# Diagonal values and state decays of three units move from GpSimd to ScalarE, and three transposes change their step

## The chip, the cores and the metric

The kernel runs on one core of a Trainium2 chip. The metric is the device time of one execution in microseconds (us), and less is better. The kernel has five instruction streams of its own: TensorE (PE), VectorE (DVE), ScalarE (ACT), GpSimd (POOL) and SyncE (SP), which issues all DMAs. Every stream runs in program order, and the streams meet at semaphores only.

## What is computed

Three layers follow one another on the tensors of four sequences (B = 4) of 768 tokens and eight heads of 48 values:

```python
# 1. attention with a decaying state
for t in range(S):
    cur = np.einsum('bhd,bhe->bhde', u[None] * kt, vt)
    y[:, :, t] = np.einsum('bhd,bhde->bhe', rt, state + cur)
    state = wt[:, :, :, None] * state + np.einsum('bhd,bhe->bhde', kt, vt)
# 2. gated MLP, 384 -> 2048 -> 384
h = x @ w_in
g = h * np.clip(h + 3.0, 0.0, 6.0) / 6.0
x = g @ w_out
# 3. soft mixture of 8 experts with 4 slots each
logits = x @ phi
d = softmax of logits over the tokens; slot_input = d.T @ x
slot_out = max(slot_input @ w1, 0) @ w2, for each expert
out = (softmax of logits over the slots) @ slot_out
```

The term `u * k * v * r` of a token with itself is the diagonal: for each head, the sum of r·u·k over its 48 values is one number for each token, and the token's v is multiplied by it.

## The kernel before

**Units and steps.** The attention is cut into 24 units: unit n is block n // 4 of 128 tokens of sequence n % 4. Units are counted from zero. The MLP is cut into 96 steps: step s = 16 g + i computes the hidden tile i (128 of the 2048 hidden values) for group g of 512 tokens (one block of all four sequences). Units 0 to 3 are computed before step 0. From then on the loop `for s in range(END)` stands in each of the five streams, and four steps go with one unit: `unit_of(s)` gives the unit n and the phase 0 to 3 of step s. Step 4 is phase 3 of unit 5, step 8 phase 3 of unit 6, step 12 phase 3 of unit 7.

**One MLP step.** TensorE multiplies the tile (nine matmuls, lines 617 to 619) into one of two PSUM banks. ScalarE makes the relu (line 1474) and VectorE the gated tile (`gate`, line 1076) and its transpose (`turn_gated`, line 1097), which goes into a ring buffer. Step s of TensorE waits for the gated tile of step s - 2, as it overwrites its bank. Every four gated tiles, TensorE adds their logits (line 665). After 16 of them, the logits of a group are folded (`low_logits` on VectorE, line 1105, then lines 696 and 697 on TensorE), their maximum is taken (line 1111), ScalarE makes weights of them (line 1499), VectorE turns these (line 1142), and in phase 2 of i = 3 of the next group TensorE gathers the slots from the ring (`gather_slots`, line 728). VectorE adds these to the accumulator at i = 4 (`add_slots`, line 1166). `turn_logits(g)` (line 1120, four small transposes) copies the folded logits of group g to the place where they are needed near the end.

**One unit.** Phase 0: TensorE makes the scores (line 501); GpSimd multiplies r, k and u (lines 1641, 1643); VectorE finishes y of the unit before (`finish_y`, line 1036, which adds the diagonal values) and adds to its state (line 1045). Phase 1: TensorE turns x (line 600); VectorE masks the scores (line 1017), then scans the decays of the next unit (lines 985, 997, and 963, 976 from unit 8 on); ScalarE splits the masked scores (`high_scores`, line 1381) and GpSimd makes their low half (`low_scores`, line 1676). Phase 2: VectorE makes the low half of x (line 1049), sums the diagonal (line 1056) and, for units 4 to 7, makes the low half of v (`low_v`, line 1060). Phase 3: TensorE computes y of the unit (`attend`; its first matmul has line 576 for units 4 to 7), which waits for the low halves of scores, v and x and for the decayed state. For units 8 and up, GpSimd makes the low half of v, and ScalarE decays the state (`decay_new_state`, line 1410).

**What the change touches.** `diag_values(n)` on GpSimd (line 1670) multiplies v by the diagonal, after it come `decay_state(n + 1)` (line 1712, for units 4 to 7) and `low_state` (line 1705). Both signal others: `finish_y` of the unit waits for `diag_v_done`, `attend` for `decayed`. In steps 1, 2, 5, 6, 9 and 10 GpSimd also makes low halves of w_in (`low_w`, line 1655), for which ScalarE makes the high half and a scaled copy (lines 1446 and 1452) in steps 0, 4, 5, 8 and 9, behind the relu of the step.

Of the kernel before, what the change touches and what calls it, by code (L numbers as in the profile page):

```python
# [50 lines left out]
def build_program(nc, wT, rkT, nat_in_dram, u, u_blocks, w_in, w_outT, w_out, phi, w1, w2, out):  # L51
    with ExitStack() as ctx:
# [900 lines left out]
        def _(dve):  # L953
# [269 lines left out]
            for s in range(END):  # L1223
                n, phase = unit_of(s)
                g, i = divmod(s, FT)
                if s <= 1:
                    gate(s)
                    if s == 0:
                        low_v(B)
                    turn_gated(s)  # L1230
                if phase == 0:
                    if 1 <= g < C and i == 1:
                        low_logits(g - 1)
                    if is_unit(n - 1):
                        finish_y(n - 1)
                    if n - 1 < LAST_INC:
                        add_state(n - 1)
                    if 1 <= g < C - 2 and i == 9:
                        turn_logits(g - 1)
                if phase == 1:  # L1240
                    if 1 <= g < C and i == 2:
                        group_maximum(g - 1)
                    if is_unit(n):
                        mask_scores(n)
                    if n + 1 < SPLIT:
                        scan_suffix(n + 1)
                        restart_prefix(n + 1)
                    elif is_unit(n + 1):
                        open_prefix(n + 1)
                        restart_suffix(n + 1)  # L1250
                    if is_unit(n - 1) and n % B == 0 and n > B:
                        low_x(n - 1)
                    if 1 <= g < C and i == 2:
                        if g == C - 1:
                            turn_gated(s - 1)
                        turn_weight(g - 1)
                    if g == C and i == 2:
                        last_maximum()
                if phase == 2:
                    if g == C and i == 3:  # L1260
                        turn_weight(C - 1)
                    if g >= 1 and i == 3:
                        sum_weight(g - 1)
                    if is_unit(n - 1) and n % B:
                        low_x(n - 1)
                    if is_unit(n):
                        sum_diag(n)
                    if n < SPLIT:
                        low_v(n)
                if s == 0:  # L1270
                    sum_diag(B)
                    low_w(1)
                if phase == 3:
                    if B < n and n + 1 < SPLIT:
                        scan_prefix(n + 1)
                    elif B < n and is_unit(n + 1):
                        close_suffix(n + 1)
                    if s == STEPS + 4:
                        dve.wait_ge(run_sum_done, C)
                        nc.vector.tensor_scalar(run_sum, run_sum, 1e-9, None, ALU.add).then_inc(sum_inv_step, 1)  # L1280
                        dve.wait_ge(sum_inv_step, 1)
                        nc.vector.reciprocal(run_sum, run_sum).then_inc(sum_inv_step, 1)
                        dve.wait_ge(sum_inv_step, 2)
                        nc.vector.tensor_scalar(fold_inv[:], fold32, run_sum, None, ALU.mult).then_inc(fold_inv_done, 1)
                        dve.wait_ge(fold_inv_done, 1)
                        nc.vector.tensor_scalar(fold_alpha, fold_inv[:], alpha, None, ALU.mult).then_inc(fold_inv_done, 1)
                    if 1 <= g < C and i == 4:
                        if g == C - 1:
                            turn_logits(g - 1)
                        add_slots(g - 1)  # L1290
                if s == 4:
                    dve.wait_ge(w_phi_ready, 4)
                    nc.vector.transpose(w_phi[:], l_ps[:]).then_inc(w_phi_done, 1)
                if s == STEPS - 12:
                    cols, tiles = c_parts[0]
                    dve.wait_ge(logits_done, C - 1)
                    nc.vector.tensor_reduce(cmax[:, tiles], by_slot(soft[:, cols]), AX_X, ALU.max).then_inc(c_max_done, 1)
                if s == STEPS - 8:
                    c_inverse(0)
                if s == STEPS + 3:  # L1300
                    copy_cT(1)
                    copy_cT(0)
                if 1 < s < STEPS - 1:
                    gate(s)
                if s == STEPS - FT - 1:
                    turn_logits(C - 3)
                if 1 < s < STEPS - 2 and s != STEPS - FT + 1:
                    turn_gated(s)
                if s == STEPS - 1:
                    last_gate(0)  # L1310
                    turn_gated(STEPS - 2)
                    last_gate(1)
                    turn_gated(STEPS - 1)
# [52 lines left out]
        def _(act):  # L1366
# [38 lines left out]
            def decay_new_state(n):  # L1405
                act.wait_ge(decay_saved, n - SPLIT + 1)
                act.wait_ge(state_added, n - B + 1)
                for p in range(PB):
                    s = state[n % B][0:PD, p, :]
                    last = nc.scalar.activation(s, s, ACT.Copy, scale=chunk_decay[n % B][0:PD, p:p + 1])  # L1410
                last.then_inc(decayed, 1)

            def high_receptance(n):
                act.wait_ge(r_dec_done, n + 1)
# [3 lines left out]
            def high_state(n):  # L1418
                if n < SPLIT:
                    act.wait_ge(state_added, n - B + 1)  # L1420
                else:
                    act.wait_ge(decayed, n - B + 1)
                    act.wait_ge(y_ready, n + 1)
                nc.scalar.activation(state_hi[n % B][0:PD], state[n % B][0:PD], ACT.Copy).then_inc(state_hi_done, 1)
# [129 lines left out]
            for s in range(END):  # L1554
                n, phase = unit_of(s)
                g, i = divmod(s, FT)
                if phase == 0:
                    if g >= 1 and i == 1:
                        copy_logit_parts(g - 1)
                    if is_unit(n):  # L1560
                        high_v(n)
                        if n >= SPLIT:
                            high_receptance(n)
                if phase == 1:
                    if is_unit(n - 1):
                        high_x(n - 1)
                    if 1 <= g < C and i == 2:
                        weigh(g - 1)
                        copy_folded(g - 1)
                    if is_unit(n):  # L1570
                        high_scores(n)
                if phase == 2:
                    if n < LAST_INC:
                        copy_keys(n)
                    if SPLIT <= n + 1 < UNITS:
                        save_decay(n + 1)
                    if SPLIT - B <= n - 2 < LAST_INC:
                        high_state(n - 2)
                if phase == 3 and SPLIT <= n - 1 < LAST_INC:
                    decay_new_state(n - 1)  # L1580
                if s < STEPS - 1:
                    relu_step(s)
                elif s == STEPS - 1:
                    for half in range(2):
                        last_relu(half)
                if s == 0:
                    copy_keys(B)
                c = scaled_behind(s)
                if c is not None:
                    high_w(c)  # L1590
                    scale_w(c)
                if g == C and i == 2:
                    weigh(C - 1)
                    copy_logits(C - 1)
                if s == STEPS - 10:
                    c_exp(0)
                if s == STEPS - 5:
                    c_high(0)
# [35 lines left out]
        def _(pool):  # L1634
# [110 lines left out]
            for s in range(END):  # L1745
# [15 lines left out]
                if phase == 3:  # L1761
                    if B < n and n + 1 < SPLIT:
                        decay_receptance(n + 1)
                    elif B < n and n + 1 < UNITS:
                        decay_keys(n + 1)
                    if is_unit(n) and n > B:
                        diag_values(n)
                    if n + 1 < SPLIT:
                        decay_state(n + 1)
                    if SPLIT - B <= n - 2 < LAST_INC:  # L1770
                        low_state(n - 2)
                c = split_behind(s)
# [75 lines left out]
```

## Time and profile before

| | |
|---|---|
| median of three runs | 410.31 us (410.25 to 410.34) |
| the profiled execution | 410.12 us, of which the span from first to last instruction is 408.4 us |
| mean granted TensorE clock | 0.992 of full speed |
| MLP steps 0 to 95 | from 35.7 us to some 352 us of the span |

The times of all rows are counted from the start of the span. In a timeline each row is one or several instructions: its start, its duration, engine, line, operation, what it writes and reads, the shape and how many; in square brackets how long the engine stood idle before and which instruction ended that. TensorE's instructions are pipelined, so a row of 0.38 us is followed by the next after 0.22 us.

### The profile page before, as it was taken

The numbers are of one execution on the slowest core, as the hardware profiler recorded it, in microseconds if no ns is written. First come the engines' busy times: TensorE is split into PE (matmuls) and PEld (weight loads), VectorE is DVE, ScalarE is ACT, GpSimd is POOL, SyncE is SP. The second block draws the span as 40 slices with busy tenths as digits, with TensorE's granted clock in tenths as the row PEclk, the third lists the DMA queues.
The fourth block names the chain that finished last, engine by engine and source line by source line (L and its number), as shares of the span: only waits on it lengthen the run. The fifth ranks groups of instructions, "written<-read, shape, count | busy, mean of one in ns | idle before, by whom it ended". The sixth has DMA issues, their size and how long they took to land.

```text
span 408.4 us, 10082 instructions
## 1 busy us (share of the span) xinstructions
PE 391.8 (96%) x3977; PEld 210.4 (52%) x3977; DVE 330.9 (81%) x536; ACT 199.8 (49%) x413; POOL 217.5 (53%) x206
## 2 busy tenths in 40 slices
PE   8999999999999999999999999999999999999981
PEld 3885555555555555555554555455543444543430
DVE  7998799998989898998989998989877886661251
ACT  3576356545555657365555646653443234321141
POOL 2444988978568677747785677875740012010000
PEclk9999999999999999999999999999999999999996
DMA  8999413439242144214431330342007199779929
GB/s 235 332 405 324 143 31 98 125 123 362 80 127 82 48 125 129 93 38 125 126 103 28 127 117 24 114 128 59 2 2 309 21 414 400 240 285 414 388 113 354
DMA packets 16542, 69.36 MB, mean 170 GB/s; under 512 B 2160, under 2 KB 3184, under 8 KB 14832
## 3 DMA queue, kind: packets, MB, share of 16 engines
q1 hardware_dynamic: 16496, 68.73, 48.6%
q8 instruction: 31, 0.51, 0.5%
q14 instruction: 15, 0.12, 0.1%
HBM read 64.00 MB, written 4.72 MB: 168 GB/s over the span
## 4 chain that ended last, share of the span: by engine, by line
PE 29%; POOL 29%; issue 27%; DMA 5%; DVE 4%; ACT 1%; SPq 1%; POOLq 0%; DVEq 0%
DMA att<-rkT_dram 5%; PE hid L617 4%; POOL att L1697 4%; PE hid L619 4%; PE hid L618 4%; POOL att L1641 4%; POOL att L1643 4%; POOL att L1670 3%; POOL att L1701 3%; POOL spare L1705 3%; PE hid L887 3%; POOL att L1662 3%; POOL w_split L1655 2%; PE inc_ps L728 1%; POOL att L1685 1%
## 5 line engine op out<-in xcount | busy, mean ns | idle before, releaser
L617 PE MATMUL hid<-x_split,w_split 128*128 128x512 f16 x285 | 108.3, 380 | 0.7 <-DVE gated L1076 0.7
L1474 ACT ACTIVATE relu<-hid,three 128x512 f32<-128x512 f32 x95 | 65.0, 684 | 88.1 <-PE hid L619 88.1
L619 PE MATMUL hid<-x_split,w_split 128*128 128x512 f16 x285 | 108.0, 379 | 0.0
L618 PE MATMUL hid<-x_split,w_split 128*128 128x512 f16 x285 | 108.0, 379 | 0.0
L1076 DVE SCALAR_TENSOR_TENSOR gated<-relu,hid 128x512 f32<-128x512 f32 x95 | 64.2, 676 | 21.5 <-ACT relu L1474 21.1
L1097 DVE STREAM_TRANSPOSE ring<-gated 128x512 f32<-128x512 f32 x96 | 68.3, 711 | 3.3
L1676 POOL TENSOR_TENSOR att<-att 128x1024 f16<-128x1024 f32 x20 | 42.1, 2104 | 34.9 <-ACT att L1381 34.9
L617 PEld LDWEIGHTS hid<-x_split,w_split 128*128 128x128 f16 x285 | 27.7, 97 | 37.1 <-issue 7.1
L619 PEld LDWEIGHTS hid<-x_split,w_split 128*128 128x128 f16 x285 | 27.8, 98 | 33.7
L1685 POOL TENSOR_TENSOR att<-att 112x512 f32<-112x512 f32 x21 | 25.5, 1213 | 36.5 <-DVE att L976 26.9
L618 PEld LDWEIGHTS hid<-x_split,w_split 128*128 128x128 f16 x285 | 27.9, 98 | 24.7
L1430 ACT ACTIVATE x_split<-y_ps 128x384 f16<-128x384 f32 x24 | 11.8, 490 | 39.8 <-PE y_ps L600 39.8
L501 PEld LDWEIGHTS sc_ps<-att 48*128 48x128 f32 x384 | 23.3, 187 | 9.3 <-issue 7.0
L501 PE MATMUL sc_ps<-att 48*128 48x128 f32 x384 | 27.9, 284 | 0.0
L1381 ACT ACTIVATE att<-att 128x1024 f16<-128x1024 f32 x20 | 21.1, 1056 | 12.6 <-DVE att L1017 11.6
L728 PE MATMUL sc_ps<-ring,soft 32*32 32x512 f32 x384 | 26.1, 598 | 0.0
L728 PE MATMUL k_ps<-ring,soft 32*32 32x512 f32 x192 | 25.7, 598 | 0.0
L1697 POOL TENSOR_TENSOR att<-att 112x512 f32<-112x512 f32 x19 | 23.5, 1235 | 3.0 <-DVE att L997 3.0
L1017 DVE TENSOR_TENSOR att<-sc_ps,mask 128x1024 f32<-128x1024 f32 x19 | 22.7, 1194 | 0.5 <-issue 0.5
L963 DVE TENSOR_TENSOR_SCAN att<-att 112x517 f32<-112x517 f32 x16 | 22.2, 1388 | 0.0
L1643 POOL TENSOR_TENSOR att<-att 128x384 f32<-128x384 f32 x20 | 20.9, 1043 | 1.6
L665 PE MATMUL l_ps<-gated,w_phi 128*32 128x512 f32 x160 | 21.3, 605 | 0.0
(300 smaller groups left out, 862.3 us busy)
## 6 DMA issues: line engine op xcount, KB each, us to landing
att<-nat_dram SPq DMA_DIRECT2D x20, 576.0 KB, 4.3
att<-rkT_dram SPq DMA_DIRECT2D x22, 448.0 KB, 5.7
att<-wT_dram SPq DMA_DIRECT2D x22, 226.2 KB, 4.7
att<-w_dram SPq DMA_DIRECT2D x3, 1536.0 KB, 9.7
out_dram<-w_split SPq DMA_DIRECT2D x11, 384.0 KB, 3.9
att<-w_dram SPq DMA_DIRECT2D x5, 768.0 KB, 10.5
stage<-w_in_dram SPq DMA_DIRECT2D x2, 1536.0 KB, 14.6
ring<-w_outT_dram SPq DMA_DIRECT2D x1, 3072.0 KB, 16.6
```

The lines of the kernel that those rows point to most:

```text
L501: last = pe.matmul(sc_bank[j][:, cols], k_dec[n % 2][rows, cols], r_dec_of(n)[rows, cols], start=True, stop=True)
L617: pe.matmul(hid[s % 2][:], high, x_high, start=(q == 0), stop=False)
L618: pe.matmul(hid[s % 2][:], high, x_low, start=False, stop=False)
L619: last = pe.matmul(hid[s % 2][:], low, x_high, start=False, stop=(q == KT - 1))
L728: ins = pe.matmul(dg_bank_of(g, a)[SLOTS * c:SLOTS * (c + 1), :], weight_T[SLOTS * a:SLOTS * (a + 1), b * SLOTS:(b + 1) * SLOTS], ring_gro ...
L1076: nc.vector.scalar_tensor_tensor(gated_tile(s), relu_tile(s), 6.0 * GATE, hid[s % 2][:], ALU.min, ALU.mult).then_inc(gated_done, 1)
L1097: nc.vector.transpose(ring_tile(s), gated_tile(s)).then_inc(gated_turned, 1)
L1474: nc.scalar.activation(relu_tile(s), hid[s % 2][:], ACT.Relu, bias=three[:], scale=GATE / H_SCALE)\
L1643: nc.gpsimd.tensor_tensor(rku, rku, u_all, ALU.mult).then_inc(rku_done, 1)
L1676: nc.gpsimd.tensor_tensor(scores_lo, scores, scores_hi, ALU.subtract).then_inc(scores_lo_done, 1)
L1685: nc.gpsimd.tensor_tensor(dst, keys, decay, ALU.mult).then_inc(k_dec_done, 1)
L1697: nc.gpsimd.tensor_tensor(dst, receptance, decay, ALU.mult).then_inc(r_dec_done, 1)
```

## The change

ScalarE gets two functions. `decay_old_state(n)` multiplies the state by the decay in four instructions, one for each pair of heads; it stands ahead of the relu of steps 0, 4 and 8, for units 5, 6 and 7. `loop_diag_values(n)` makes the diagonal values in eight instructions, one for each head; it stands behind the relu of steps 4, 8 and 12, for units 5, 6 and 7. GpSimd no longer does either for these units, one instruction each. Unit 4 stays on GpSimd, and the diagonal values of units 8 and up as well.

On VectorE three things move. `turn_logits(2)` runs in step 53 instead of step 57. `turn_gated(80)` runs at its place behind `gate(80)` no more, but in step 82, where `turn_gated(81)` stood; `turn_gated(81)` runs at the head of phase 2 of step 83.

```diff
@@ VectorE
-                    if 1 <= g < C - 2 and i == 9:
+                    if (g, i) in ((1, 9), (2, 9), (3, 5)):
                         turn_logits(g - 1)
...
                     if 1 <= g < C and i == 2:
                         if g == C - 1:
-                            turn_gated(s - 1)
+                            turn_gated(s - 2)
                         turn_weight(g - 1)
...
                 if phase == 2:
+                    if s == STEPS - FT + 3:
+                        turn_gated(s - 2)
...
-                if 1 < s < STEPS - 2 and s != STEPS - FT + 1:
+                if 1 < s < STEPS - 2 and s not in (STEPS - FT, STEPS - FT + 1):
                     turn_gated(s)
@@ ScalarE
+            def decay_old_state(n):
+                act.wait_ge(suffix_done, n + 1)
+                act.wait_ge(state_copied, n - B + 1)
+                for p in range(PB):
+                    s = state[n % B][0:PD, p, :]
+                    first = 1 + p * (P + 1)
+                    last = nc.scalar.activation(s, s, ACT.Copy, scale=suffix[0:PD, first:first + 1])
+                last.then_inc(decayed, 1)
+
+            def loop_diag_values(n):
+                act.wait_ge(diag_done, n + 1)
+                act.wait_ge(y_done, n)
+                if n >= SPLIT:
+                    act.wait_ge(v_scaled, n - SPLIT + 1)
+                for h in range(H):
+                    cols = slice(h * D, (h + 1) * D)
+                    last = nc.scalar.activation(diag_v[:, cols], nat_of(n, 2)[:, cols], ACT.Copy, scale=diag[:, h:h + 1])
+                last.then_inc(diag_v_done, 1)
...
+                if phase == 3 and n + 1 < SPLIT:
+                    decay_old_state(n + 1)
                 if phase == 3 and SPLIT <= n - 1 < LAST_INC:
                     decay_new_state(n - 1)
                 if s < STEPS - 1:
...
                 if s == 0:
                     copy_keys(B)
+                if phase == 3 and B < n < SPLIT:
+                    loop_diag_values(n)
@@ GpSimd
-                    if is_unit(n) and n > B:
+                    if is_unit(n) and n >= SPLIT:
                         diag_values(n)
-                    if n + 1 < SPLIT:
-                        decay_state(n + 1)
```

## Rows read from the trace of the kernel before

**Rows 1.** The page, part 1: busy time, share and instructions.

```profile
PE 391.8 (96%) x3977; PEld 210.4 (52%) x3977; DVE 330.9 (81%) x536; ACT 199.8 (49%) x413; POOL 217.5 (53%) x206
```

**Rows 2.** The waits: who waited for whom; us, times, longest.

```profile
DVE att L1036 <- POOL att L1670: 7.5, 11, 0.8
```

**Rows 3.** The timeline of TensorE, steps 4, 8 and 12 with their attends.

```profile
52.79 0.39 PE L617 MATMUL hid<-x_split,w_split 128*128 128x512 f16 x1
...
56.40 0.38 PE L617 MATMUL hid<-x_split,w_split 128*128 128x512 f16 x1
...
68.46 0.43 PE L576 MATMUL y_ps<-att 112*128 112x96 f32 x2 [0.47 <-DVE att L1060]
...
80.00 0.38 PE L617 MATMUL hid<-x_split,w_split 128*128 128x512 f16 x1 [0.27 <-DVE gated L1076]
...
83.11 0.43 PE L576 MATMUL y_ps<-att 112*128 112x96 f32 x2 [1.01 <-DVE att L1060]
...
84.83 0.38 PE L617 MATMUL hid<-x_split,w_split 128*128 128x512 f16 x1
```

**Rows 4.** The timeline of VectorE, steps 5 to 12, and a scan of step 22.

```profile
59.89 0.68 DVE L1076 SCALAR_TENSOR_TENSOR gated<-relu,hid 128x512 f32<-128x512 f32 x1
...
62.35 2.05 DVE L985 TENSOR_TENSOR_SCAN att<-att 112x517 f32<-112x517 f32 x1
...
66.76 1.44 DVE L1060 SCALAR_TENSOR_TENSOR att<-att 128x384 f16<-128x384 f32 x1
...
72.79 0.56 DVE L1036 SCALAR_TENSOR_TENSOR att<-y_ps,att 128x384 f32<-128x384 f32 x1 [0.81 <-POOL att L1670]
...
73.72 0.68 DVE L1076 SCALAR_TENSOR_TENSOR gated<-relu,hid 128x512 f32<-128x512 f32 x1
...
76.32 2.73 DVE L963 TENSOR_TENSOR_SCAN att<-att 112x517 f32<-112x517 f32 x1
...
79.18 0.67 DVE L1076 SCALAR_TENSOR_TENSOR gated<-relu,hid 128x512 f32<-128x512 f32 x1
...
120.30 1.21 DVE L963 TENSOR_TENSOR_SCAN att<-att 112x517 f32<-112x517 f32 x1
```

**Rows 5.** ScalarE: two groups by line and shape, relus of steps 5 and 9, split scores.

```profile
L1410 ACT ACTIVATE att<-att,stats 112x96 f32<-112x96 f32 x48 | 14.0, 372 | 0.0
L1469 ACT ACTIVATE att<-soft,diag 128x48 f32<-128x48 f32 x8 | 1.9, 323 | 0.0
...
58.54 0.69 ACT L1474 ACTIVATE relu<-hid,three 128x512 f32<-128x512 f32 x1 [0.89 <-PE hid L619]
...
72.33 0.69 ACT L1474 ACTIVATE relu<-hid,three 128x512 f32<-128x512 f32 x1 [1.59 <-PE hid L619]
...
76.30 1.06 ACT L1381 ACTIVATE att<-att 128x1024 f16<-128x1024 f32 x1 [0.92 <-DVE att L1017]
```

**Rows 6.** GpSimd: a group by line and shape, then the low scores of unit 7.

```profile
L1670 POOL TENSOR_TENSOR att<-att,diag 128x384 f32<-128x384 f32 x20 | 16.6, 828 | 0.1
...
77.91 2.93 POOL L1676 TENSOR_TENSOR att<-att 128x1024 f16<-128x1024 f32 x1
```

**Rows 7.** Timelines of TensorE (steps 81, 86) and VectorE (step 84).

```profile
315.71 0.38 PE L696 MATMUL l_ps<-soft,fold 128*128 128x512 f16 x1 [0.41 <-DVE soft L1105]
...
329.53 0.39 PE L617 MATMUL hid<-x_split,w_split 128*128 128x512 f16 x1
...
324.93 0.87 DVE L1166 SCALAR_TENSOR_TENSOR acc<-acc,stats,inc_ps 128x384 f32<-128x384 f32 x2 [0.60 <-PE k_ps L728]
...
328.80 0.68 DVE L1076 SCALAR_TENSOR_TENSOR gated<-relu,hid 128x512 f32<-128x512 f32 x1
```

**Rows 8.** Timelines, steps 56 and 57: keys decayed, scores, logits turned.

```profile
238.03 1.19 POOL L1685 TENSOR_TENSOR att<-att 112x512 f32<-112x512 f32 x1 [1.79 <-DVE att L976]
...
240.29 1.16 PE L501 MATMUL sc_ps<-att 48*128 48x128 f32 x16
...
241.03 1.25 DVE L1120 STREAM_TRANSPOSE logits<-soft 32x128 f32<-32x128 f32 x4
```

## The prediction, made before the change was run

> **What bounds the kernel now.** Start with the busy shares [rows 1]: TensorE is busy for 96% of the span, GpSimd for 53% and ScalarE for 49%. So relief for GpSimd is worth nothing by itself. It counts only where TensorE stands idle on a chain that runs through GpSimd. The list of waits names one such place [rows 2]: `finish_y` on VectorE waits for the diagonal values 11 times, 7.5 us in all. That VectorE waits is no loss yet; TensorE has to wait for VectorE in turn. So go on to TensorE's timeline, and there to the three attends of units 5, 6 and 7, the only units whose diagonal values move [rows 3]. Unit 5 runs without a gap: from the start of step 4 (52.79) to that of step 5 (56.40) are 3.61 us, which is nine matmuls and the attend. Before the attend of unit 6 stands an idle 0.47 us (start 68.46), before step 12 one of 0.27 us (80.00), and before the attend of unit 7 one of 1.01 us (83.11). Step 12 takes 84.83 - 80.00 = 4.83 us, 1.22 more than step 4. The whole prize of the first part is therefore at most 0.47 + 0.27 + 1.22 = 1.96 us, some 2.2 if a restart at step 8 costs as much beyond its idle time as at step 12. All three gaps end on VectorE: on `low_v` (line 1060) twice, on `gate` once.
>
> Now VectorE [rows 4]. Its chain ahead of those gaps has three things in it that can shrink. `finish_y` of unit 6 waited 0.81 us for GpSimd (72.79). The scan of decays at 62.35 took 2.05 us and that at 76.32 took 2.73 us, while the same scan in step 22 took 1.21. And `low_v` took 1.44 us at 66.76. The slow scan at 76.32 runs while GpSimd makes low halves, the last of them the low scores from 77.91 on, itself slow at 2.93 us [rows 6]. I take it that the two engines hold each other up.
>
> The Trainium skill says so too: "GPSIMD Engine Reference", section "Specifications", lists the SBUF interfaces as shared with VectorE, with contention for VectorE instructions with two SBUF inputs. The scans and `low_v` are such, `gate` (one input from PSUM) is not, and the gate at 79.18 shows its usual 0.67 us [rows 4]. By that rule the slowdown goes only where the overlap goes, which is what the sum below does from rows.
>
> **Part 1, what moves to ScalarE.** GpSimd loses three instructions of 0.83 us (line 1670) [rows 6] and three of line 1712 over as many columns, which I take at the same 0.83, in each unit between a decay of k or r and the products of the next unit, so its later work in steps 5 to 10 can start 1.6 us sooner. ScalarE gets 12 small instructions for each. The eight of line 1469 are the same work (128x48, a scale for each partition): mean 323 ns each, 1.9 us for eight [rows 5]. The row gives the group's union, so they do overlap; unoverlapped they would be 8 x 0.323 = 2.6. The four state decays have their twin in line 1410: 372 ns each, at most 1.5 us for four. The decays stand ahead of the relus of steps 0, 4 and 8, where in steps 4 and 8 ScalarE waits for TensorE's tile anyway, so I cost them at nothing; in step 0 they push the relu by about 1 us, and TensorE next needs that tile in step 2. If this cover were gone, 1.2 to 1.5 us would come on the relu. `decayed` is signalled steps before the attend reads it.
>
> The diagonal values stand behind the relu of step s, and queued behind them are the pieces of w_in, v of the next unit and the relu of step s + 1. That relu is the price. In step 5 it started at 58.54 after 0.89 us idle [rows 5], so ScalarE was free at 57.65; with 1.9 us more it is free at 59.55, the relu ends at 60.24, and `gate` of step 5, at 59.89 before [rows 4], comes at 60.3, 0.4 late. In step 9 ScalarE was free at 72.33 - 1.59 = 70.74, now at 72.64; the relu ends at 73.33.
>
> What comes of it at unit 6: the masks of scores follow the gate, 0.4 us late, and so do ScalarE's split scores and GpSimd's low scores. The scan at 62.35 starts at 62.75, but GpSimd's piece of w_in has gone 1.6 us sooner, and it runs nearly alone: 1.2 to 1.3 us in place of 2.05. It ends at 64.0 in place of 64.4. The gate behind it then waits for the relu that is 0.4 late, and comes at 64.55 or so; `low_v` at 66.76 stays, its overlap too. **The gap at 68.46 stays; I book 0**, between +0.4 (late relu, no gain on `low_v`) and -0.7 (1.44 falls to 0.7, the width of a free pass).
>
> At unit 7: `finish_y` no longer waits, and VectorE arrives 0.81 us sooner, at 71.98; then the gate of step 9 waits for its relu until 73.35, where it came at 73.72. So everything from here is 0.37 us early: the scan starts at 75.95. GpSimd's low scores, at 77.91 before because GpSimd was busy, now wait for the split scores alone (76.30 + 1.06 - 0.37 [rows 5]), until some 77.05. The scan shares 0.35 us with the piece of w_in ahead of them, which ended at 77.9 and now ends at 76.3 (at half pace, as 2.73 against 1.21 says: 0.17 done), runs alone for 0.75 and has 0.29 left at half pace, 0.58. That is 1.7 us in place of 2.73, and an end at 77.65 in place of 79.05. The gate at 79.18 comes 1.4 sooner, `low_v` follows it in VectorE's queue and keeps its length, and the attend starts at 81.7 in place of 83.11. **Gain 1.4 us**; bounds 0.4 (the scan keeps 2.73) and 1.5 (the gaps at 80.00 and 83.11 are all gone). What is late next is `low_v` still, by some 0.1 us.
>
> The Trainium skill speaks against this part: "ScalarE: Activation LUTs", section "Rules for kernel authors", wants multiplications on VectorE rather than ScalarE, and its section "What ACT_TABLE_LOAD costs" gives each instruction 186 ns, 93 more with a pointer operand, before the first element. An estimate from that page is 319 ns for 48 values. The 323 ns of the row agree. One instruction of GpSimd becomes eight with eight fixed costs; by the rule the diagonal values cost ScalarE more than they save GpSimd (1.9 against 0.83 us), which is the second rival.
>
> **Part 2, `turn_logits(2)` in step 53.** It is four transposes, 1.25 us [rows 8]. In step 53 it pushes the masks of unit 18, so the split scores, so the relu of step 54, and VectorE is 0.8 to 0.9 us late until the scan that the keys' decay waits for. This decay ran 238.03 to 239.22, and TensorE's scores need it at 240.29: 1.07 us of room [rows 8], which is used up nearly but not quite. In step 57 the 1.25 us are missing, and VectorE is ahead again. There was no gap of TensorE to close at either place. I book +0.05, between 0 and 0.4.
>
> **Part 3, the gated tiles.** Without `turn_gated(80)`, 0.64 us, `low_logits` comes sooner, and the fold at 315.71 loses its wait of 0.41 [rows 7] and starts about 0.56 sooner. So does the gather of step 83. But the turn is added again in step 83, on VectorE, ahead of `add_slots`, whose idle 0.60 us (324.93) it fills exactly. The gate of step 84 at 328.80 [rows 7] stands behind `add_slots` and stays where it is, perhaps 0.04 later. TensorE's step 86 started at 329.53, 0.05 after this gate's end, and must wait for it. So what TensorE wins in step 81 it waits for in front of step 86; as it then restarts from idle, a little is lost. I book +0.1, between -0.56 (the gate doesn't bind) and +0.2.
>
> **The sum.** 0 - 1.4 + 0.05 + 0.1 = -1.25 us on the profiled execution's 410.12, which gives 408.9. This execution is 0.2 below the median of 410.31, so the median would come at 409.06, and I say 409.0. From step 13 on the steps repeat a pattern that TensorE sets, and no transfer of that stretch goes by the clock, so I expect the gain to stay to the end. The forecast's own range is 408.3 to 409.49. Anything within 0.2% (0.82 us) can't be told from no change for this kernel.
>
> **The rivals.**
> - *The overlap stays.* If the scan at 76.32 keeps its 2.73 us because GpSimd's work only shifts along with it, the gain is the 0.37 us of the gate in step 9: 410.31 - 0.37 + 0.15 = 410.1. For it: low scores and scan both hang on the same masks. Against it: the low scores also need ScalarE's split of 1.06 us first. That the gain is some 0.7 rather lies here too. Chance 0.24.
> - *ScalarE becomes late.* Mechanism: the eight instructions in front of the relu of step 5. It decides as soon as the late gate costs more than the freed scan gives (0.85 us). If they don't overlap (2.6 us) the gate comes 1.1 late, and `low_v` and the attend of unit 6 0.7 to 1.1 later; at unit 7 the later relu eats the 0.4. That gives 410.31 + 0.9 + 0.15 = 411.4, slower. Against it: the group's 1.9 us [rows 5]. Chance 0.10.
> - *Step 86 isn't bound by its gate.* Then the 0.56 us of part 3 stay: 409.0 - 0.1 - 0.56 = 408.3. For it: 0.05 us between that gate and the matmul is short for a wait. Chance 0.12.
> - *Nothing arrives*, since the late relus take what `finish_y` gives: 410.3. Chance 0.04.
>
> **How the numbers follow.** The forecast keeps 0.50. Faster by over 0.2% are forecast and third rival, 0.62, and 0.02 of the first; within 0.2% the rest of the first and the fourth, 0.26; slower 0.10. The range leaves out the slow rival and little else: 408.1 to 410.4.
>
> **What would show it.** In the profile after: ScalarE's rows of the new functions at 1.9 us and at 1.2 to 1.5 us; the relus of steps 5 and 9 later by 0.9 and 0.3; no wait of `finish_y` for GpSimd in steps 9 and 13; the scan of unit 8 at 1.7 us; the gap before unit 7's attend under 0.2 us with that before unit 6's near 0.5; a fold of step 81 without a wait, and step 86 waiting for its gate. I am wrong if the scans keep their lengths, if the gap of unit 6 grows, or if a gap opens behind step 53.

## The result

| | before | after |
|---|---|---|
| median of six runs | 410.28 us (410.12 to 410.34) | 408.07 us (407.66 to 409.22) |
| span of the profiled execution | 408.4 us | 406.3 us |
| start of step 13 | 84.83 | 83.20 |
| start of step 64 | 259.79 | 257.68 |
| start of step 82 | 316.14 | 313.46 |
| start of step 86 | 329.53 | 327.45 |

The ratio is 0.9952 (95% interval 0.9938 to 0.9967), so 1.4 to 2.5 us came off. The forecast was 409.0, with a range from 408.1 to 410.4: the direction was right, the size too small by nearly 1 us, and the median lies 0.03 us under the range's low end (by the ratio, 408.3 us, it lies inside). The profiled execution of the changed kernel took 409.01 us, 2.7 of them outside its span; in four of the six runs 1.7 to 1.9 us lie there. So from here on the spans and the starts of steps are compared. A start is that of the step's first matmul (line 617).

Of the new functions, `decay_old_state` has line 1421 and `loop_diag_values` line 1431. The relu is line 1495 now, and the lines of GpSimd lie 25 further down (1676 is 1701). First the busy times and what `finish_y` waited, from the page and the list of waits of the changed kernel; it answers to [rows 1, 2].

```profile
PE 391.6 (96%) x3977; PEld 210.1 (52%) x3977; DVE 329.2 (81%) x536; ACT 208.1 (51%) x449; POOL 210.5 (52%) x200
...
DVE att L1036 <- POOL att L1695: 5.3, 7, 0.8
```

ScalarE has 8.3 us more and GpSimd 7.0 less, of which six instructions of 0.83 us are 5.0; most of the rest is that two of its low scores became 0.59 and 0.93 us shorter. TensorE does the same work in 2.1 us less span. Four waits of `finish_y` for the diagonal values are gone: those of units 5 to 7, and one more, of unit 4. Next TensorE's timeline of the changed kernel, which answers to [rows 3]; the first row is the attend of unit 4.

```profile
42.67 0.43 PE L576 MATMUL y_ps<-att 112*128 112x96 f32 x2 [0.80 <-DVE att L1060]
...
68.29 0.43 PE L576 MATMUL y_ps<-att 112*128 112x96 f32 x2
...
79.49 0.39 PE L617 MATMUL hid<-x_split,w_split 128*128 128x512 f16 x1
...
81.47 0.43 PE L576 MATMUL y_ps<-att 112*128 112x96 f32 x2
...
83.20 0.38 PE L617 MATMUL hid<-x_split,w_split 128*128 128x512 f16 x1
```

All three gaps of units 6 and 7 are closed; none of their rows has an idle time. Step 12 takes 3.71 us in place of 4.83. But the attend of unit 4, in step 1, waits 0.80 us, and step 2 started 0.23 us later than before. VectorE's timeline of the changed kernel answers to [rows 4]:

```profile
40.71 1.71 DVE L1060 SCALAR_TENSOR_TENSOR att<-att 128x384 f16<-128x384 f32 x1
...
60.30 0.69 DVE L1076 SCALAR_TENSOR_TENSOR gated<-relu,hid 128x512 f32<-128x512 f32 x1 [0.43 <-ACT relu L1495]
...
62.77 1.22 DVE L985 TENSOR_TENSOR_SCAN att<-att 112x517 f32<-112x517 f32 x1
...
66.80 1.23 DVE L1060 SCALAR_TENSOR_TENSOR att<-att 128x384 f16<-128x384 f32 x1
...
71.74 0.52 DVE L1036 SCALAR_TENSOR_TENSOR att<-y_ps,att 128x384 f32<-128x384 f32 x1
...
73.48 0.69 DVE L1076 SCALAR_TENSOR_TENSOR gated<-relu,hid 128x512 f32<-128x512 f32 x1 [0.76 <-ACT relu L1495]
...
76.09 1.24 DVE L963 TENSOR_TENSOR_SCAN att<-att 112x517 f32<-112x517 f32 x1
...
77.73 0.69 DVE L1076 SCALAR_TENSOR_TENSOR gated<-relu,hid 128x512 f32<-128x512 f32 x1 [0.19 <-ACT relu L1495]
```

The two scans take 1.22 and 1.24 us where they took 2.05 and 2.73. Where `finish_y` waited for GpSimd, the gates of steps 5 and 9 now wait for their relus, 0.43 and 0.76 us. ScalarE and GpSimd show why, and answer to [rows 5, 6]: the new instructions, the relus behind them, and on GpSimd a piece of w_in and the low scores of unit 7.

```profile
38.34 1.16 ACT L1421 ACTIVATE att<-att 112x96 f32<-112x96 f32 x4
...
55.77 1.91 ACT L1431 ACTIVATE att<-att,diag 128x48 f32<-128x48 f32 x8
...
59.60 0.67 ACT L1495 ACTIVATE relu<-hid,three 128x512 f32<-128x512 f32 x1
...
72.78 0.67 ACT L1495 ACTIVATE relu<-hid,three 128x512 f32<-128x512 f32 x1
...
74.58 1.65 POOL L1680 TENSOR_TENSOR w_split<-stage,w_split 128x768 f16<-128x768 f32 x1
...
77.20 2.00 POOL L1701 TENSOR_TENSOR att<-att 128x1024 f16<-128x1024 f32 x1 [0.97 <-ACT att L1383]
```

The scan from 76.09 to 77.33 falls almost whole into the hole of GpSimd between 76.23 and 77.20. Last the two other places, which answer to [rows 7, 8]. A row of the kernel before first, which the prediction had not read, then the changed kernel: TensorE at steps 64, 81 and 86, VectorE in steps 83 and 84.

```profile
259.79 0.38 PE L617 MATMUL hid<-x_split,w_split 128*128 128x512 f16 x1 [0.44 <-DVE gated L1076]
```

```profile
257.68 0.38 PE L617 MATMUL hid<-x_split,w_split 128*128 128x512 f16 x1
...
313.02 0.38 PE L696 MATMUL l_ps<-soft,fold 128*128 128x512 f16 x1
...
327.45 0.39 PE L617 MATMUL hid<-x_split,w_split 128*128 128x512 f16 x1 [0.26 <-DVE gated L1076]
...
318.21 1.31 DVE L1097 STREAM_TRANSPOSE ring<-gated 128x512 f32<-128x512 f32 x2
...
322.85 0.87 DVE L1166 SCALAR_TENSOR_TENSOR acc<-acc,stats,inc_ps 128x384 f32<-128x384 f32 x2
...
326.71 0.68 DVE L1076 SCALAR_TENSOR_TENSOR gated<-relu,hid 128x512 f32<-128x512 f32 x1
```

Step 64 had a gap of 0.44 us in the kernel before, and has none now. The fold of step 81 has lost its wait. Step 86 has got one of 0.26 us, for the gate of step 84, in front of which two turns stand in one row (318.21) and `add_slots` without its idle time (322.85).

### The profile page after: what moved, and what is told of

It is laid out like the page before. It is cut to its first block, busy times and chain, and to the rows that moved or that the text cites. A ratio compares the mean times of both kernels' runs of the same rounds, so it can differ in the third digit from the quotient of the medians.

```text
span 406.3 us, 10112 instructions
## 1 busy us (share of the span) xinstructions
PE 391.6 (96%) x3977; PEld 210.1 (52%) x3977; DVE 329.2 (81%) x536; ACT 208.1 (51%) x449; POOL 210.5 (52%) x200
## 4 chain that ended last, share of the span: by engine, by line
PE 74%; DVE 10%; issue 6%; ACT 5%; DMA 2%; POOL 0%; SPq 0%; DVEq 0%; POOLq 0%; ACTq 0%
PE hid L617 13%; PE hid L619 12%; PE hid L618 12%; PE l_ps L665 5%; PE sc_ps L501 4%; PE l_ps L728 3%; PE hid L887 3%; PE inc_ps L530 2%; PE y_ps L600 2%; DVE gated L1076 1%; ACT relu L1495 1%; PE hid L868 1%; PE k_ps L511 1%; PE sc_ps L868 1%; PE y_ps L576 1%
## 5 line engine op out<-in xcount | busy, mean ns | idle before, releaser
L1495 ACT ACTIVATE relu<-hid,three 128x512 f32<-128x512 f32 x95 | 65.1, 685 | 82.2 <-PE hid L619 81.7
L1701 POOL TENSOR_TENSOR att<-att 128x1024 f16<-128x1024 f32 x20 | 40.2, 2011 | 39.7 <-ACT att L1383 39.7
L589 PE MATMUL y_ps<-att 128*128 128x48 f16 x160 | 21.0, 185 | 0.0
```

The lines of the kernel that those rows point to most:

```text
L1495: nc.scalar.activation(relu_tile(s), hid[s % 2][:], ACT.Relu, bias=three[:], scale=GATE / H_SCALE)\
L1701: nc.gpsimd.tensor_tensor(scores_lo, scores, scores_hi, ALU.subtract).then_inc(scores_lo_done, 1)
```

## The experiments

The starts of steps, as a difference to the kernel before in us, tell the parts apart. Each is from one profiled execution. The stretch up to step 2 varies by some tenths from execution to execution: the kernel of e3 lost 0.74 us in step 1, where it does the same as the kernel before. So a stretch is read as the difference of two entries of its column.

| start of step | before | after | e1 | e2 | e3 | e4 | e5 | e6 | e7 | e10 | e8 | e9 |
|---|---|---|---|---|---|---|---|---|---|---|---|---|
| 0 | 35.72 | +0.02 | +0.08 | +0.23 | +0.03 | +0.08 | +0.01 | +0.03 | -0.12 | +0.06 | -0.04 | +0.19 |
| 2 | 46.35 | +0.23 | +0.28 | +0.24 | +0.77 | +0.08 | +0.01 | +0.24 | +0.08 | +0.06 | +0.17 | +0.19 |
| 9 | 70.19 | -0.17 | -0.12 | +0.26 | +0.77 | -0.33 | -0.40 | -0.36 | +0.36 | +0.07 | -0.25 | -0.23 |
| 13 | 84.83 | -1.64 | -1.67 | +0.27 | +0.79 | -1.88 | -1.15 | -1.12 | -1.00 | +0.08 | -1.72 | -1.76 |
| 17 | 98.47 | -1.63 | -1.67 | +0.28 | +0.80 | -1.88 | -1.14 | -1.11 | -0.24 | +0.08 | -1.71 | -1.76 |
| 63 | 257.25 | -1.63 | -1.66 | +0.28 | +0.80 | -1.88 | -1.14 | -1.12 | -0.25 | +0.08 | -1.73 | -1.75 |
| 64 | 259.79 | -2.12 | -1.68 | -0.24 | +0.79 | -2.38 | -1.14 | -1.13 | -0.25 | +0.21 | -2.25 | -2.27 |
| 82 | 316.14 | -2.68 | -1.69 | -0.22 | +0.21 | -2.95 | -1.15 | -1.10 | -0.25 | +0.20 | -2.79 | -2.81 |
| 86 | 329.53 | -2.08 | -1.69 | -0.22 | +0.81 | -2.35 | -1.15 | -1.11 | -0.25 | +0.20 | -2.79 | -2.81 |

### e1: part 1 alone

```diff
-                    if (g, i) in ((1, 9), (2, 9), (3, 5)):
+                    if 1 <= g < C - 2 and i == 9:
...
-                    if s == STEPS - FT + 3:
-                        turn_gated(s - 2)
```

(with the other two lines of part 3 as in the kernel before)

> Part 1 alone: ScalarE makes the diagonal values and decays of units 5 to 7, and the three transposes stay where they were. Measured for the whole change: step 13 starts 1.64 us sooner, and steps 63 and 64 bring another 0.49 us. Theory (the 0.49 us is part 2's): the 1.64 us come back, the 0.49 us do not; the span is 408.4 - 1.64 = 406.8 us and the start of step 64 is 1.63 us sooner than before. Rival (the 0.49 us follow from VectorE being earlier after part 1): step 64 is 2.12 us sooner and the span 406.3 us.

Measured: 408.67 us (ratio 0.995, 0.9922 to 0.9978), span 406.7. Step 13 is 1.67 us sooner, and step 64 no more than that. The rival is out: the 0.49 us at step 64 do not follow from part 1. Its TensorE still waits there:

```profile
258.11 0.38 PE L617 MATMUL hid<-x_split,w_split 128*128 128x512 f16 x1 [0.42 <-DVE gated L1076]
```

### e2: part 2 alone

```diff
-                    if 1 <= g < C - 2 and i == 9:
+                    if (g, i) in ((1, 9), (2, 9), (3, 5)):
```

> Part 2 alone: turn_logits(2) in step 53 instead of 57. Theory: TensorE's step 64 waits for the gate of step 62, at the end of a VectorE chain that turn_logits in step 57 delays; without it step 64 comes 0.49 us sooner and stays so: span 407.9 us. The prediction's view (VectorE's lateness reached no gap of TensorE) and the rival of the first run: no change or up to 0.4 us later, span 408.4 to 408.8 us.

Measured: 409.88 us (0.9976, 0.9945 to 1.0006), which alone would not settle it. The steps do: from +0.28 at step 63 to -0.24 at step 64, 0.52 us gained in one step, and not a hundredth of a microsecond lost between steps 53 and 63. Its span of 408.4 us is that of the kernel before because this execution began 0.23 us late and another 0.2 us came on behind step 86. The prediction's view is out.

### e10: the same transposes in step 61

```diff
-                    if 1 <= g < C - 2 and i == 9:
+                    if (g, i) in ((1, 9), (2, 9), (3, 13)):
```

> The kernel before with turn_logits(2) in step 61 instead of 57, so nearer to step 64. Theory (step 64 waits for the gate of step 62 at the end of a VectorE chain): all its 1.25 us are on that chain now, where in step 57 only 0.49 us of them arrived; step 64 starts 0.5 to 0.9 us later than in the kernel before, and keeps that to the end. Rival (step 64 is late for another reason and step 57's transposes only met a tight spot there): step 64 comes 0.49 us sooner, as with step 53.

Measured: 410.38 us (0.9995, 0.9973 to 1.0017); step 64 0.13 us later. The rival is out, as nothing was gained. But the size expected (0.5 to 0.9) was wrong. Read TensorE, then VectorE of this kernel; the kernel before had `finish_y` of unit 19 at 253.47 and its scan (line 963) of 1.52 us at 256.87:

```profile
260.00 0.38 PE L617 MATMUL hid<-x_split,w_split 128*128 128x512 f16 x1 [0.58 <-DVE gated L1076]
...
252.71 0.56 DVE L1036 SCALAR_TENSOR_TENSOR att<-y_ps,att 128x384 f32<-128x384 f32 x1 [0.61 <-POOL att L1689]
253.19 0.55 DVE L1045 TENSOR_TENSOR att<-att,inc_ps 112x384 f32<-112x384 f32 x1
253.65 1.24 DVE L1120 STREAM_TRANSPOSE logits<-soft 32x128 f32<-32x128 f32 x4
...
257.38 1.22 DVE L963 TENSOR_TENSOR_SCAN att<-att 112x517 f32<-112x517 f32 x1
...
259.18 0.68 DVE L1076 SCALAR_TENSOR_TENSOR gated<-relu,hid 128x512 f32<-128x512 f32 x1
```

VectorE arrives 0.76 us sooner since step 57 is free of the transposes, has them now (1.25), and its scan is 0.30 us shorter: -0.76 + 1.25 - 0.30 = 0.19, against 0.21 us of the gate of step 62 (259.18 for 258.97). The chain is as supposed; step 61 costs only 0.13 us more than step 57, as most of a delay in step 57 reaches step 64 too.

### e3: part 3 alone

```diff
-                            turn_gated(s - 1)
+                            turn_gated(s - 2)
...
+                    if s == STEPS - FT + 3:
+                        turn_gated(s - 2)
...
-                if 1 < s < STEPS - 2 and s != STEPS - FT + 1:
+                if 1 < s < STEPS - 2 and s not in (STEPS - FT, STEPS - FT + 1):
```

> Part 3 alone: turn_gated(80) in step 82, turn_gated(81) in step 83. Theory as predicted: the fold of step 81 and steps 82 to 85 come 0.56 us sooner, step 86 waits for its gate and is where it was or 0.05 us later: span 408.4 us. Rival (step 86 bound by TensorE): span 407.85 us.

Measured: 410.37 us (0.9984, 0.9959 to 1.0009). From step 81 to 82 TensorE wins 0.57 us and before step 86 it gives 0.60 back, so part 3 by itself costs 0.03 us. The span of 409.2 holds the 0.74 us lost in step 1; that start is not part 3's doing, as no instruction before step 80 differs.

### e8: the turn where VectorE waits

```diff
                         low_logits(g - 1)
+                        if g == C - 1:
+                            turn_gated(s - 1)
...
-                            turn_gated(s - 2)
+                            turn_gated(s - 1)
...
-                    if s == STEPS - FT + 3:
-                        turn_gated(s - 2)
```

> The whole change, but turn_gated(80) stands right behind low_logits in step 81, where VectorE waits 1.22 us for a relu, and turn_gated(81) stays in step 82 as in the kernel before. Theory (part 3's 0.56 us are given back because the turn in step 83 delays add_slots and so the gate of step 84): step 82 comes 0.56 us sooner as with the change, add_slots starts 0.5 to 0.6 us sooner than with the change, and step 86 keeps the gain: 0.5 to 0.65 us sooner than with the change, span 405.7 us. Rival (step 86 is held by something else in that stretch): step 86 stays where it was, span 406.3 us.

Measured: 407.57 us (0.9929, 0.9915 to 0.9943), span 405.6. Step 86 is 0.71 us sooner than with the change, of which 0.11 were there at step 82, so the 0.60 us are kept. VectorE's timeline of this kernel: the turn at 312.54 leaves 0.61 of the 1.22 us wait, and `add_slots` starts at 322.14 in place of 322.85.

```profile
312.54 0.69 DVE L1097 STREAM_TRANSPOSE ring<-gated 128x512 f32<-128x512 f32 x1
313.84 0.69 DVE L1076 SCALAR_TENSOR_TENSOR gated<-relu,hid 128x512 f32<-128x512 f32 x1 [0.61 <-ACT relu L1495]
...
322.14 0.87 DVE L1166 SCALAR_TENSOR_TENSOR acc<-acc,stats,inc_ps 128x384 f32<-128x384 f32 x2
```

### e4: the decay of unit 5 back on GpSimd

```diff
-                if phase == 3 and n + 1 < SPLIT:
+                if phase == 3 and B < n and n + 1 < SPLIT:
                     decay_old_state(n + 1)
...
+                    if n == B:
+                        decay_state(n + 1)
```

> The whole change, but the decay of unit 5 is GpSimd's again, in step 0. With the change, four decays ahead of the relu of step 0 made the gate and low_v of unit 4 later, and TensorE's step 2 came 0.23, step 5 0.33 us later than before. Theory: those 0.33 us are the price of this placement, and VectorE, which bounds units 6 and 7, gets them as well: the start of step 13 is 0.2 to 0.33 us sooner than with the change, span 406.0 us. Rival: GpSimd's 0.83 us ahead of the products of unit 5 cost as much, and the span is 406.3 us or more.

Measured: 407.73 us (0.9921, 0.9894 to 0.9949), span 406.0. Steps 1 to 8 lose nothing now, and step 13 is 1.88 + 0.08 = 1.96 us sooner as counted from step 0, in place of 1.66: the decays ahead of the relu of step 0 cost 0.30 us. (Against e1, which lost 0.21 us at step 2 as well but not the 0.10 at step 5, it is 0.21; so the price is 0.2 to 0.3.) 1.96 is also the whole prize that the prediction counted. The attend of unit 4 waits again as in the kernel before:

```profile
42.53 0.43 PE L576 MATMUL y_ps<-att 112*128 112x96 f32 x2 [0.59 <-POOL att L1701]
```

### e5 and e6: the halves of part 1

e5 leaves `decay_old_state` out and keeps GpSimd's `decay_state`; e6 leaves `loop_diag_values` out and keeps GpSimd's `diag_values`. Parts 2 and 3 are undone in both.

```diff
-                if phase == 3 and n + 1 < SPLIT:
-                    decay_old_state(n + 1)
```

> Half of part 1: ScalarE makes the diagonal values of units 5 to 7, GpSimd keeps all decays of the state; parts 2 and 3 undone. No four decays stand ahead of the relu of step 0, so steps 2 to 8 start as before. GpSimd is ahead by 0.8 us for each unit, not 1.6. Theory (VectorE's wait for the diagonal values and the overlap each count): at unit 7 the wait of 0.81 us is gone, but the piece of w_in on GpSimd ends at some 77.1 instead of 76.3 and runs beside the scan of unit 8, which takes 1.9 to 2.2 us; step 13 starts 0.9 to 1.4 us sooner. Rival (only the wait counts): step 13 is 1.6 us or more sooner, as with all of part 1.

```diff
-                if phase == 3 and B < n < SPLIT:
-                    loop_diag_values(n)
```

> The other half of part 1: ScalarE decays the states of units 5 to 7, GpSimd keeps all diagonal values; parts 2 and 3 undone. The diagonal values stand ahead of the decays on GpSimd, so finish_y waits as before. Theory: what is left is GpSimd's 0.8 us in each unit for the overlap, less the 0.3 us that the decays ahead of the relu of step 0 cost: step 13 is 0 to 0.7 us sooner. Rival (the decays on GpSimd are the main cost): 1 us or more sooner.

Measured: e5 409.38 us (0.9974, 0.9948 to 1.0), step 13 1.16 us sooner counted from step 0; e6 409.6 us (0.9953, 0.9919 to 0.9988), step 13 1.15 us sooner, although it pays for step 0 too. For e5 the theory held: its scan takes 2.15 us. For e6 it failed: `finish_y` still waits its 0.81 us, and yet 1.15 us came. That is the rival's number, but not for the rival's reason, since e5 gained as much with the decays still on GpSimd. VectorE of e5 (the first row), then of e6:

```profile
75.75 2.15 DVE L963 TENSOR_TENSOR_SCAN att<-att 112x517 f32<-112x517 f32 x1
```

```profile
72.43 0.56 DVE L1036 SCALAR_TENSOR_TENSOR att<-y_ps,att 128x384 f32<-128x384 f32 x1 [0.81 <-POOL att L1691]
...
75.97 1.97 DVE L963 TENSOR_TENSOR_SCAN att<-att 112x517 f32<-112x517 f32 x1
```

So the wait for the diagonal values was not a price in itself. GpSimd's diagonal values follow its decay of r, this follows a scan on VectorE, and the scan follows `low_v`. Shorten VectorE's work ahead of them, and the wait stays 0.81 but stands sooner (72.43 for 72.79). Either half gives GpSimd 0.8 us for each unit, and with it two thirds of the gain; the second half gives the rest only. The halves don't add up because the gaps to be closed hold 1.96 us, no more.

### e7: GpSimd kept busy

```diff
+            def pad(n):
+                pool.wait_ge(diag_done, n + 1)
+                nc.gpsimd.tensor_tensor(pairs(rku, D), pairs(u_all, D),
+                                        diag[:].rearrange("p (h o) -> p h o", o=1).broadcast_to([P, H, D]),
+                                        ALU.mult).then_inc(padded, 1)
...
+                    if B < n < SPLIT:
+                        pad(n)
+                    if n + 1 < SPLIT:
+                        pad(n)
```

> Part 1 alone, but GpSimd does in place of each instruction that it gave up one of the same length whose result nobody uses (it multiplies u by the diagonal into the products' tile, and waits for itself), so finish_y no longer waits and GpSimd is as busy as before. Theory (the larger part of part 1 is the overlap of GpSimd's work with the scan): the scan of unit 8 keeps 2.2 to 2.8 us, and step 13 starts only 0 to 0.6 us sooner than before. Rival (the wait of finish_y is what counts): the scan's length does not matter and step 13 is 1.6 us sooner, as with part 1.

Measured: 410.08 us (0.999, 0.9963 to 1.0017). Step 13 is 0.88 us sooner counted from step 0, step 17 only 0.12. The gain of e1 is 1.75 by the same count, so some 1.6 us of it hang on GpSimd's free time; all else that part 1 does, late relus included, is worth 0.1 net. Not all of the 1.6 is the length of the scans: 0.87 us were missing at step 13, and 0.76 went in step 13 itself. (Two pads take 1.74 us where two instructions took 1.62, so the load is slightly over that of before.) VectorE, GpSimd and TensorE of this kernel, whose lines are one higher on VectorE and TensorE:

```profile
62.61 2.14 DVE L986 TENSOR_TENSOR_SCAN att<-att 112x517 f32<-112x517 f32 x1
...
76.00 2.04 DVE L964 TENSOR_TENSOR_SCAN att<-att 112x517 f32<-112x517 f32 x1
...
76.91 2.57 POOL L1679 TENSOR_TENSOR w_split<-stage,w_split 128x768 f16<-128x768 f32 x1
...
86.62 1.16 PE L502 MATMUL sc_ps<-att 48*128 48x128 f32 x16 [0.68 <-POOL att L1719]
```

Both scans are slow again, and the piece of w_in beside the second takes 2.57 us in place of 1.65. The expectation of 2.2 to 2.8 us for the scan was a little high, since GpSimd's products fell beside its head. That the last 0.76 us go in step 13, where the scores wait for the keys' decay on GpSimd, was not expected: there TensorE was bound by GpSimd's queue, and the pads, 0.12 us longer than what they stand for, can have a small part in it.

### e9: both repairs

e9 is the changed kernel with the edits of e4 and of e8.

> Both repairs at once: the decay of unit 5 is GpSimd's again (e4), turn_gated(80) behind low_logits (e8). The stretches lie 300 us apart, so the gains add up: 0.25 to 0.3 and 0.55 to 0.6 us off the changed kernel's span of 406.3, which gives 405.4 us, and a median of 407.2 us; ratio to the kernel before 0.9925. Rival (a shift of TensorE's early steps opens a new gap later): 406 us or more.

Measured: 407.37 us, ratio 0.9931 to the kernel before (0.9918 to 0.9945), span 405.5 in an execution that began 0.19 us late. Counted from step 0, step 86 is 3.00 us sooner than before, against 2.75 in e8 and 2.10 with the change. The gains add up. By the medians it lies 0.2 us under e8 and 0.7 under the changed kernel; the first of these is within what single runs scatter, and only the steps show it.

## Why the prediction was nearly right

**Part 1, unit 7: the chain and the end were right, the length of the scan was not.** Forecast: the attend at 81.7, the gate of step 10 at 77.78, the scan 1.7 us. Measured: 81.47, 77.73, 1.24. The scan was oversized for two reasons. The piece of w_in ended at 76.23, 0.14 us after the scan's start in place of 0.35, and the low scores came only at 77.20. And "at half pace" is not what the rows show: the scan waits for the piece of w_in that started first, and the low scores, starting second, would have held nothing up (see the last section). With the forecast's own times that gives 1.4 to 1.5 us, not 1.7. The shorter scan brought nothing beyond the forecast, as the gate then waited 0.19 us for its relu. `low_v` at 1.23 in place of 1.44 made the rest. The relus of steps 5 and 9 came at 59.60 and 72.78 (forecast 59.55 and 72.64), and the gate of step 5 at 60.30, as forecast.

**Part 1, unit 6: booked 0, and 0.17 us came at step 9.** The gate of step 6 came at 64.55 as forecast; `low_v`, forecast at 66.76 with 1.44 us, came at 66.80 with 1.23, so it ended 0.17 us sooner. The gap vanished for another reason as well: TensorE was 0.33 us late when it came there.

**Step 0 was booked at nothing, and that was wrong.** The step that failed is "TensorE next needs that tile in step 2". It looked at the tile alone. Behind the gate of step 0, VectorE's queue holds `low_v` of unit 4, for which the attend in step 1 waits. It ended at 42.42, as it started 0.98 us later than before and took 1.71 us in place of 0.72, behind low scores that had started first, at 40.01. The cost was 0.21 us at step 2 and another 0.10 at step 5; e4 puts the whole at 0.30 us, or 0.21 against e1. So part 1 came near its forecast partly by luck: it closed gaps of 1.96 us where 1.4 were booked, and paid 0.30 where nothing was booked.

**Part 2: booked +0.05, measured -0.49 to -0.52.** The cost side was right: nothing was lost behind step 53. The step that failed is the sentence "There was no gap of TensorE to close at either place". There was one, 0.44 us, seven steps on, at the first step of the next group. Steps 62 and 63 are short for TensorE, because units from 20 on need neither keys turned nor an increment (1.94 us in place of 2.33 for step 58, and 2.06 with the gap closed in place of 2.63 for step 59), and VectorE's scans, gates and turns go on as before. So TensorE catches up with VectorE there, and what delays VectorE in step 57 is paid in step 64. e1, e2 and e10 show it. This term makes over half of what the forecast missed.

**Part 3: as forecast.** 0.56 us sooner at the fold, and 0.60 to 0.61 us given back before step 86, by the idle 0.60 us that the added turn fills. The forecast had 0.04 us for the gate and took it for 0.1 on TensorE; the measured sum is +0.04 with the change and +0.03 alone.

**The rivals.** *The overlap stays* did not come, but e7 shows that it was the right thing to fear: with GpSimd as busy as before, 0.12 us are left, though only part of the loss is the scans' length. *ScalarE becomes late* did not come; the eight instructions took 1.91 us, and the freed scans gave more than the 0.4 us late gate took. *Step 86 isn't bound by its gate* is out by e3 and e8. *Nothing arrives* is out by the 1.75 us of e1. Of the signs, the gap before unit 6's attend, expected near 0.5 us, is gone; and the 0.9 us for the relu of step 5 should read 1.0 by the prediction's own working (1.06 came). The rule of the Trainium skill against multiplications on ScalarE ("ScalarE: Activation LUTs", section "Rules for kernel authors") compares ScalarE with VectorE, and no run here put this work on VectorE. Against GpSimd, which the rule does not speak of, the price was 1.91 us for eight instructions in place of 0.83 for one, of which ScalarE's idle time took up 0.85 us in step 5 and 1.46 in step 9, so that the relus came only 1.06 and 0.45 us later.

The sum, by terms: part 1 -1.4 forecast, -1.66 measured; part 2 +0.05 and -0.49; part 3 +0.1 and +0.04; together -1.25 and -2.10 us, counted from step 0.

## What to carry to other kernels

Before a wait is called harmless, list every gap of the engine that bounds the kernel, over its whole length and not only near the change: a delay on the second engine can lie hidden for seven steps and be paid where the first engine's work gets short. When an instruction is put in front of another, follow the queues of the engines that wait for the latter, not the one result that it makes. And a piece of work that is moved away from a busy stretch belongs where its engine waits anyway; moved to another busy stretch it only moves the bill. Where two engines hold each other up, look at which instruction starts first, not only at how much they overlap.

## What the runs showed of the hardware

VectorE and GpSimd hold each other up, and which one pays is decided by which instruction starts first. The scan of 112x517 values took 1.21 to 1.25 us alone or nearly so, 1.97 to 2.15 in the shared rows above, and 2.73 at worst. GpSimd's low scores took 2.00 us alone and 2.93 at worst, its piece of w_in 1.65 and 2.57. Put the start times beside these. First GpSimd's piece of w_in in the kernel before, 0.02 us ahead of the scan at 76.32; then GpSimd in e5, around the scan at 75.75:

```profile
76.30 1.66 POOL L1655 TENSOR_TENSOR w_split<-stage,w_split 128x768 f16<-128x768 f32 x1
```

```profile
75.15 1.66 POOL L1676 TENSOR_TENSOR w_split<-stage,w_split 128x768 f16<-128x768 f32 x1
76.86 2.83 POOL L1697 TENSOR_TENSOR att<-att 128x1024 f16<-128x1024 f32 x1
```

The instruction that started first kept its length, and the other grew by nearly all the time that the first still had to run. In the kernel before, the piece of w_in had 1.64 us left and the scan grew by 1.52; then the low scores came second, the scan had 1.14 left, and they grew by 0.93. In e5 1.06 left made 0.94, and 1.04 left made 0.83. In e7, where the products of GpSimd ran first (0.95 us left), the scan at 76.00 grew by 0.83, and the piece of w_in behind it, second this time, by 0.92 of the scan's 1.13. So the rows do not show two engines at half pace, but the later one held for nearly as long as the earlier one still runs. This is read from start times, and no run was made for it alone. It also says what the change did at unit 7: there GpSimd's piece of w_in is all but done when the scan starts, and the scan all but done when the low scores start.

`gate`, with one input in PSUM, took 0.65 to 0.69 us in all these rows. "GPSIMD Engine Reference" of the Trainium skill, section "Specifications", names instructions of VectorE with two SBUF inputs, and these rows agree. What had not been expected is the size: freed from 1.6 us of GpSimd's work per unit, VectorE's two scans became 0.83 and 1.49 us shorter.
